# Channel attention and a gated feed-forward: steps of 1024 tokens (and one of 896 per batch) in place of 752

## The chip, the cores and the metric

The kernel runs on one core of one Trainium2 chip. The metric is the device time of one execution in microseconds; the median of several runs is compared.

## The reference

Two computations in sequence, all in float32. `q`, `k` and `v` have the shape (2, 6016, 256), `w_in` (256, 2048), `w_out` (2048, 256).

```
qn = q / (norm(q, axis=1) + 1e-06);  kn = k / (norm(k, axis=1) + 1e-06)
s = kn.transpose(0, 2, 1) @ qn / tau          # 256 x 256 for each batch
a = softmax(s, axis=-1)
x = v @ a                                     # 12032 tokens x 256
h = x @ w_in
g = h * (1.0 / (1.0 + exp(-h)))
out = g @ w_out
```

## The kernel before

**Head.** For each batch, 47 rows of 128 tokens of `q` and `k` are loaded in chunks of up to 3 rows into a ring of 9 slots (`load_chunk`, L222; two of the slots lie in `wp_raw0`, L118). PE sums the scores of all tokens (`score_chunk`, L336), ACT squares and DVE adds the squares (L503, L680), `sum_norms` (L341) sums them over the partitions. Softmax gives `probs`. Then `fold` (L359) multiplies `probs` into `w_in` once for each batch, so that the tokens of `v` go through one folded matrix to the hidden layer.

**Two-part numbers.** Every matrix factor is held as a rounded part and its rest (`_hi`, `_lo`, type float32r), and a product is three matmuls: hi by hi, hi by lo, lo by hi (`product`, L370, lines 373 to 375; `output_part`, L405, lines 408 to 410; `fold`, lines 365 to 367).

**Steps.** The tokens of a batch are cut into 8 steps of 2 x 376 (TOK = 376), 16 steps in all. The hidden layer of a step is a 2 x 2 block product for each of 8 pairs of 128-wide blocks of `d_ff`, done with 7 products in place of 8: factors A12, A22, A11 and the sums S1 to S4 of the folded matrix, and B11, B21, B22 with the sums T1 to T4 of the token halves. A pair is 7 x 3 product matmuls and 8 x 3 output matmuls, 45 in all, each over TOK columns. PE's order within a pair is written out by hand (`step`, L433): four first products (P1, P6, P5, P7), the first outputs of the pair before, three last products (P2, P3, P4), the last outputs of the pair before. Between them ACT copies P1 into `u` (L575), DVE adds the partial sums (L773, L777, L780, L792, L794), ACT applies silu (L588, L591, L601) and rounds (L595, L560), DVE subtracts for the rests (L796, L766). All of these cover TOK or 2 x TOK elements of each partition. Each engine works its list strictly in order and waits on semaphores.

**Tokens of the next step.** SP loads four blocks of `v` into `v_raw` (`load_v`, L232) once the split of the step before is over (`next_v`, L264). DVE makes T1 to T4 into `t_raw` after pairs 1 to 3 (`sum_v`, L739), ACT rounds B in pair 2 and T in pair 4 (L551, L555), DVE splits after pairs 4 to 6 (`split_v`, L752). `b_hi` and `b_lo` are double buffers. For step 0 POOL makes the sums and splits during the head (L307 to L321).

**Factors.** In step 0, PE also folds the second batch into `wp_raw1` (in pair 0, four folds after the first products, four after the last), and ACT and DVE round and split the factors of the first batch two pairs ahead (`round_a`, `sum_a`, `split_a`). The last step of batch 0 and the first of batch 1 replace them by those of batch 1 (`reloading`, L786 to L789).

**Outputs.** They are summed over the 8 pairs in four PSUM banks. ACT copies them in pair 0 of the next step into `out_sb`, a tile of its own (`copy_out`, L562), after the store of the step before has landed; SP stores each half (`store`, L258), and its order alternates stores and loads:

```
                    store(2 * it + half - 1)
                    next_v(0, 2 * it + half)
```

## Time and profile before

| | |
|---|---|
| median of 3 runs | 1106.34 us (1106.28 to 1107.59) |
| profiled execution, its own time | 1107.88 us |
| its span, first to last instruction | 1106.1 us |
| mean granted TensorE clock | 1.000 |
| busy: PE, DVE, ACT, POOL | 99%, 67%, 58%, 3% |
| step matmuls | 5760 of 376 columns |

The profile is one execution. PE is TensorE's matmuls, PEld its weight loads, DVE VectorE, ACT ScalarE, POOL GpSimd, SP the engine that issues most transfers. Matmuls are pipelined and the profile models their ends, so what one matmul costs is read from start to start. A row such as L373 names the line of the kernel printed above.

### The profile page before, as it was taken

The page shows a single profiled execution, that of the slowest core. Times are in us where ns is not written, and L with a number is a line of the kernel's source. Part 1 is how long each engine was busy: PE and PEld are TensorE (multiplying, and loading weights), DVE is VectorE, ACT ScalarE, POOL GpSimd, SP SyncE. Part 2 cuts the span into 40 slices and gives each one's busy share as a digit, 9 for nine tenths or more (in the row PEclk, how much of TensorE's full clock was granted, in tenths as well). Part 3 has the DMA queues.
Part 4 walks back from the last instruction along what each step waited for, and adds up shares of the span by engine and source line. Part 5 has one row for each costly group of instructions (what it writes and reads, how often), then busy time and mean ns, then how long its engine had stood idle before and what let it go on. Part 6 is the DMA issues. An engine that isn't in the chain of part 4 may idle for free.

```text
span 1106.1 us, 16838 instructions
## 1 busy us (share of the span) xinstructions
PE 1099.7 (99%) x6264; PEld 1082.7 (98%) x6264; DVE 741.2 (67%) x1194; ACT 646.0 (58%) x977; POOL 32.4 (3%) x24
## 2 busy tenths in 40 slices
PE   9999999999999999999999999999999999999998
PEld 7888999999999999999999999999999999999998
DVE  5686796666666666666687776666666666666654
ACT  5786765555555555555565656555554655555544
POOL 2450000000000000000000000000000000000000
PEclk9999999999999999999999999999999999999999
DMA  9990001010101001010100000010100000010000
GB/s 344 394 363 1 1 1 57 1 56 1 29 29 29 28 14 42 0 56 0 31 25 28 29 29 29 1 57 1 57 1 28 28 28 28 0 56 0 28 0 28
DMA packets 30627, 54.12 MB, mean 49 GB/s; under 512 B 2928, under 2 KB 22128, under 8 KB 30576
## 3 DMA queue, kind: packets, MB, share of 16 engines
q1 hardware_dynamic: 30000, 52.83, 13.5%
q10 hardware_dynamic: 576, 0.66, 0.2%
q8 instruction: 26, 0.43, 0.2%
q14 instruction: 25, 0.20, 0.1%
HBM read 41.16 MB, written 12.32 MB: 48 GB/s over the span
## 4 chain that ended last, share of the span: by engine, by line
PE 94%; DMA 2%; ACT 2%; DVE 1%; issue 1%; SPq 0%; ACTq 0%; DVEq 0%
PE ps_o L410 16%; PE ps_o L409 16%; PE ps_o L408 16%; PE ps_h L373 14%; PE ps_h L375 14%; PE ps_h L374 14%; PE ps_o L336 3%; DMA qk<-k_dram 2%; ACT ps_h L503 1%; DVE square_sum L680 0%; PE ps_h L365 0%; PE ps_h L366 0%; PE ps_h L367 0%; PE ps_o L366 0%; PE ps_o L367 0%
## 5 line engine op out<-in xcount | busy, mean ns | idle before, releaser
L373 PE MATMUL ps_h<-b_hi,a_hi_rest 128*128 128x376 f32 x672 | 223.9, 333 | 0.0
L375 PE MATMUL ps_h<-b_hi,a_lo_rest 128*128 128x376 f32 x672 | 223.9, 333 | 0.0
L374 PE MATMUL ps_h<-b_lo,a_hi_rest 128*128 128x376 f32 x672 | 223.3, 332 | 0.0
L792 DVE TENSOR_TENSOR h_b<-ps_h,u 128x376 f32<-128x376 f32 x128 | 70.4, 550 | 164.4 <-PE ps_h L375 164.2
L410 PE MATMUL ps_o<-g_hi_b,wo_lo 128*128 128x376 f32 x512 | 171.4, 335 | 0.0
L773 DVE TENSOR_TENSOR u<-ps_h,u 128x376 f32<-128x376 f32 x128 | 70.3, 550 | 150.8 <-ACT u L575 136.6
L409 PE MATMUL ps_o<-g_lo_b,wo_hi 128*128 128x376 f32 x512 | 171.2, 334 | 0.0
L408 PE MATMUL ps_o<-g_hi_a,wo_hi 128*128 128x376 f32 x512 | 170.8, 334 | 0.0
L410 PE MATMUL ps_o<-g_hi_a,wo_lo 128*128 128x376 f32 x512 | 170.8, 334 | 0.0
L408 PE MATMUL ps_o<-g_hi_b,wo_hi 128*128 128x376 f32 x512 | 170.6, 333 | 0.0
L409 PE MATMUL ps_o<-g_lo_a,wo_hi 128*128 128x376 f32 x512 | 170.4, 333 | 0.0
L591 ACT ACTIVATE h_a<-ps_h 128x376 f32<-128x376 f32 x128 | 62.1, 485 | 150.1 <-PE ps_h L375 150.1
L601 ACT ACTIVATE h_b<-h_b 128x752 f32<-128x752 f32 x128 | 106.8, 835 | 41.3 <-DVE h_b L794 41.3
L588 ACT ACTIVATE h_a<-h_a 128x376 f32<-128x376 f32 x128 | 66.3, 518 | 107.1 <-DVE h_a L780 105.7
L575 ACT ACTIVATE u<-ps_h 128x376 f32<-128x376 f32 x128 | 62.1, 485 | 114.2 <-PE ps_h L375 114.1
L374 PEld LDWEIGHTS ps_h<-b_lo,a_hi_rest 128*128 128x128 f32 x672 | 126.5, 188 | 0.0
L375 PEld LDWEIGHTS ps_h<-b_hi,a_lo_rest 128*128 128x128 f32 x672 | 126.2, 188 | 0.0
L373 PEld LDWEIGHTS ps_h<-b_hi,a_hi_rest 128*128 128x128 f32 x672 | 126.1, 188 | 0.0
L796 DVE TENSOR_TENSOR g_lo_a<-h_a,g_hi_a 128x752 fp32r<-128x752 f32 x128 | 119.3, 932 | 1.8 <-ACT g_hi_a L595 1.8
L766 DVE TENSOR_TENSOR g_lo_b<-h_b,g_hi_b 128x752 fp32r<-128x752 f32 x128 | 119.3, 932 | 1.6 <-ACT g_hi_b L560 1.6
L595 ACT ACTIVATE g_hi_a<-h_a 128x752 fp32r<-128x752 f32 x128 | 106.8, 834 | 7.2
L560 ACT ACTIVATE g_hi_b<-h_b 128x752 fp32r<-128x752 f32 x128 | 105.7, 826 | 0.7 <-PE ps_o L410 0.7
(111 smaller groups left out, 1752.8 us busy)
## 6 DMA issues: line engine op xcount, KB each, us to landing
v_raw<-v_t_dram SPq DMA_DIRECT2D x64, 188.0 KB, 2.7
out_t_dram<-out_sb SPq DMA_DIRECT2D x30, 376.0 KB, 2.8
qk<-q_dram SPq DMA_DIRECT2D x23, 384.0 KB, 9.3
qk<-k_dram SPq DMA_DIRECT2D x23, 384.0 KB, 12.3
wp_raw<-q_dram SPq DMA_DIRECT2D x6, 384.0 KB, 9.1
wp_raw<-k_dram SPq DMA_DIRECT2D x6, 384.0 KB, 10.7
wp_raw<-w_out_dram SPq DMA_DIRECT2D x4, 512.0 KB, 12.2
wp_raw<-w_in_dram SPq DMA_DIRECT2D x4, 512.0 KB, 13.1
```

What stands on the lines that cost most here:

```text
L373: nc.tensor.matmul(ps_h[:, bank, 0:TOK], w_hi, x_hi, start=start, stop=False, skip_group_check=True)
L374: nc.tensor.matmul(ps_h[:, bank, 0:TOK], w_hi, x_lo, start=False, stop=False, skip_group_check=True)
L375: return nc.tensor.matmul(ps_h[:, bank, 0:TOK], w_lo, x_hi, start=False, stop=stop, skip_group_check=True)
L408: nc.tensor.matmul(out, wo_hi[:, block_, d], g_hi[:, i, :], start=start, stop=False)
L409: nc.tensor.matmul(out, wo_hi[:, block_, d], g_lo[:, i, :], start=False, stop=False)
L410: return nc.tensor.matmul(out, wo_lo[:, block_, d], g_hi[:, i, :], start=False, stop=stop)
L560: nc.scalar.activation(g_hi_b[:], h_b[:], ACT.Copy).then_inc(hi_b, 1)
L595: nc.scalar.activation(g_hi_a[:], h_a[:], ACT.Copy).then_inc(hi_a, 1)
L601: nc.scalar.activation(h_b[:], h_b[:], ACT.Silu).then_inc(silu_b, 1)
L766: nc.vector.tensor_tensor(g_lo_b[:], h_b[:], g_hi_b[:].bitcast(F32), ALU.subtract).then_inc(lo_b, 1)
L792: nc.vector.tensor_tensor(h_b[:, 0, :], ps_h[:, BANK_P5, 0:TOK], u[:], ALU.add).then_inc(c12_made, 1)
L796: nc.vector.tensor_tensor(g_lo_a[:], h_a[:], g_hi_a[:].bitcast(F32), ALU.subtract).then_inc(lo_a, 1)
```

## The change

The tokens of a batch go in five steps of 2 x 512 and a last one of 2 x 448 (6 steps for each batch, 12 in all). Matmuls of the last step cover 448 columns; elementwise instructions cover 512 in all steps. To hold the wider tiles: `out_sb` becomes a view of `v_raw`; T3 and T4 are written over `v_raw`'s first and third block, so `t_raw` has two blocks; `b_lo1` takes the place of `wp_raw0`, and the factor order T1 to B22 lets each part of it be written after the pairs that it covers are used up; four ring slots lie in that region; `probs` and `q_scale` move to the area shared by early and late tiles. The order on SP is now, for each step: both stores, a wait for their landing, then the load of the step after the next, written out instead of looped. `copy_out` waits for the split of the next tokens rather than for a store. Sums, roundings and splits of tokens are regrouped over pairs 2 to 6. In the head, fold 0 of the first batch is placed before `sum_norms(1)`, and its copy before the second batch's roots; ACT rounds the first tokens in three pieces. The loops of PE, ACT and DVE now run over an odd and an even step, with steps 0, 5, 6 and 11 written out.

```diff
-TOK = 376
+TOK = 512
+NARROW = 448
...
-B11, B21, B22, T1, T2, T3, T4 = range(7)
+T1, T2, T3, T4, B11, B21, B22 = range(7)
...
-    STEPS = N // (2 * TOK)
+    WIDE = N // (2 * TOK)
+    STEPS = WIDE + 1
...
+        with ExitStack() as early:
+            wp_raw = [sb("wp_raw0", [P, PAIRS, 4, P], stack=early)]
+            homes = [sb(f"home{n}", [P, slot + C], stack=early)[:, 0:slot] for n in range(2)]
+        b_lo1 = sb("b_lo1", [P, FACTORS, TOK], F32R)
+        sb("rest_of_wp_raw0", [P, (4 * PAIRS * P - FACTORS * TOK)])
...
-        t_raw = sb("t_raw", [P, 4, TOK])
+        out_sb = v_raw[:].rearrange("p (t c) n -> p t c n", c=CK)
+        t_raw = sb("t_raw", [P, 2, TOK])
         b_hi = [sb("b_hi0", [P, FACTORS, TOK], F32R)]
-        b_lo = [sb("b_lo0", [P, FACTORS, TOK], F32R)]
+        b_lo = [sb("b_lo0", [P, FACTORS, TOK], F32R), b_lo1]
...
@@ sync, load_v and the stores
-                sp.dma_start(v_raw[:, 0, :], v_halves[:, b, 0, 2 * step + 1, :]).then_inc(v_loaded, 16)
-                sp.dma_start(v_raw[:, 1, :], v_halves[:, b, 0, 2 * step, :]).then_inc(v_loaded, 16)
-                sp.dma_start(v_raw[:, 2, :], v_halves[:, b, 1, 2 * step, :]).then_inc(v_loaded, 16)
-                sp.dma_start(v_raw[:, 3, :], v_halves[:, b, 1, 2 * step + 1, :]).then_inc(v_loaded, 16)
+            def load_v(step):
+                first, n = tokens_of(step)
+                for i, (c, t) in enumerate(((0, 1), (0, 0), (1, 0), (1, 1))):
+                    sp.dma_start(v_raw[:, i, 0:n], v_t[step // STEPS, c * P:(c + 1) * P,
+                                                       first + t * n:first + (t + 1) * n]).then_inc(v_loaded, 16)
...
+            def out_half(step, t):
+                first, n = tokens_of(step)
+                first += step // STEPS * N + t * n
+                return out_t.rearrange("(c p) n -> p c n", p=P)[:, :, first:first + n]
+            for step in range(ALL - 1):
+                n = tokens_of(step)[1]
+                for late, t in enumerate((1, 0)):
+                    sp.wait_ge(out_copied, 2 * step + late + 3)
+                    sp.dma_start(out_half(step, t), out_sb[:, t, :, 0:n]).then_inc(out_stored, 16)
+                if step < ALL - 2:
+                    sp.wait_ge(out_stored, 32 * step + 64)
+                    load_v(step + 2)
+            for late, t in enumerate((1, 0)):
+                last = out_half(ALL - 1, t)
+                sp.wait_ge(last_copied_dve, late + 1)
...
@@ gpsimd, step 0: the same new order of sums and splits
...
@@ tensor
-                nc.tensor.matmul(ps_h[:, bank, 0:TOK], w_hi, x_hi, start=start, stop=False, skip_group_check=True)
...
+                x_hi, x_lo = b_hi[par][:, t, 0:n], b_lo[par][:, t, 0:n]
+                nc.tensor.matmul(ps_h[:, bank, 0:n], w_hi, x_hi, start=start, stop=False, skip_group_check=True)
+                nc.tensor.matmul(ps_h[:, bank, 0:n], w_hi, x_lo, start=False, stop=False, skip_group_check=True)
+                return nc.tensor.matmul(ps_h[:, bank, 0:n], w_lo, x_hi, start=False, stop=stop,
                                         skip_group_check=True)
-            def first_products(n, pair, par, folded=False):
+            def first_products(n, pair, par, tok, folded=False):
...
-            sum_norms(1)
             pe.wait_ge(w_in_split, PARTS)
             pe.wait_ge(probs_split, 1)
+            pe.wait_ge(chunk_added, 2 * len(CHUNKS) - 1)
             for group in range(FOLDS):
                 fold(0, group)
+                if group == 0:
+                    sum_norms(1)
...
             step(0, 0, opening=True)
-            step(1, 1)
-            with pe.Fori(1, STEPS // 2) as it:
-                step(2 * it, 0)
+            with pe.Fori(0, WIDE // 2) as it:
                 step(2 * it + 1, 1)
-            step(STEPS, 0, reloaded=True)
-            step(STEPS + 1, 1)
-            with pe.Fori(STEPS // 2 + 1, ALL // 2) as it:
-                step(2 * it, 0)
+                step(2 * it + 2, 0)
+            step(STEPS - 1, 1, tok=NARROW)
+            step(STEPS, 0, before=NARROW, reloaded=True)
+            with pe.Fori(STEPS // 2, ALL // 2 - 1) as it:
                 step(2 * it + 1, 1)
-            first_outputs(PAIRS * ALL - 1, ALL - 1, PAIRS - 1)
+                step(2 * it + 2, 0)
...
@@ scalar
+            def round_t12(it, par):
+                act.wait_ge(t12_summed, it + 1)
+                nc.scalar.activation(b_hi[par][:, T1:T2 + 1, :], t_raw[:], ACT.Copy).then_inc(t12_rounded, 1)
             def round_v(it, par):
                 act.wait_ge(v_loaded, 64 * it + 64)
-                nc.scalar.activation(b_hi[par][:, B11:B22 + 1, :], v_raw[:, 1:4, :], ACT.Copy).then_inc(v_rounded, 1)
-            def round_t(it, par):
-                act.wait_ge(v_summed, it + 1)
-                nc.scalar.activation(b_hi[par][:, T1:T4 + 1, :], t_raw[:], ACT.Copy).then_inc(v_rounded, 1)
+                nc.scalar.activation(b_hi[par][:, B11:B22 + 1, :], v_raw[:, 1:4, :], ACT.Copy).then_inc(b_rounded, 1)
+            def round_t34(it, par):
+                act.wait_ge(t4_summed, it + 1)
+                nc.scalar.activation(b_hi[par][:, T3:T4 + 1, :], v_raw[:, 0:3:2, :], ACT.Copy).then_inc(t34_rounded, 1)
             def round_b(n):
...
+                act.wait_ge(v_split, 3 * it + 6)
+                nc.scalar.activation(out_sb[:, 1], ps_o[:, CK:2 * CK, :], ACT.Copy).then_inc(out_copied, 1)
                 act.wait_ge(o2_done, PAIRS * it + PAIRS + 1)
-                nc.scalar.activation(out_sb[:, 0], ps_o[:, 0:CK, 0:TOK], ACT.Copy).then_inc(out_copied, 1)
+                nc.scalar.activation(out_sb[:, 0], ps_o[:, 0:CK, :], ACT.Copy).then_inc(out_copied, 1)
             def step(it, par, opening=False, reloading=None, closing=False):
                 for pair in range(PAIRS):
...
+                    if not closing and pair == 3:
+                        round_t12(it + 1, 1 - par)
+                    if not closing and pair == 4:
                         round_v(it + 1, 1 - par)
-                    if not closing and pair == 4:
-                        round_t(it + 1, 1 - par)
+                    if not closing and pair == 6:
+                        round_t34(it + 1, 1 - par)
                     act.wait_ge(c22_made, n + 1)
                     nc.scalar.activation(h_a[:, 0, :], h_a[:, 0, :], ACT.Silu).then_inc(silu_22, 1)
                     act.wait_ge(p2_done, n + 1)
                     act.wait_ge(lo_a, n + 1)
-                    nc.scalar.activation(h_a[:, 1, :], ps_h[:, BANK_P1, 0:TOK], ACT.Silu).then_inc(silu_11, 1)
+                    nc.scalar.activation(h_a[:, 1, :], ps_h[:, BANK_P1, :], ACT.Silu).then_inc(silu_11, 1)
                     act.wait_ge(silu_22, n + 1)
...
+                if g == SECOND + 3:
+                    round_t12(0, 0)
                 if g == SECOND + 4:
                     root_norms(0)
                 if g == SECOND + 5:
                     exponentials(0)
-                    round_t(0, 0)
+                    round_t34(0, 0)
                 if g in (25, 26, 27, 28):
                     round_w_in(g - 25)
                 if g == SECOND + 13:
                     round_probs(0)
...
@@ vector
+            def sum_t123(it):
+                dve.wait_ge(v_loaded, 64 * it + 64)
+                dve.wait_ge(v_split, 3 * it)
+                nc.vector.tensor_tensor(t_raw[:, 0, :], b12_raw, b11_raw, ALU.subtract).then_inc(v_step, 1)
+                dve.wait_ge(v_step, it + 1)
+                nc.vector.tensor_tensor(b12_raw, b22_raw, b12_raw, ALU.subtract)
+                nc.vector.tensor_tensor(t_raw[:, 1, :], b22_raw, t_raw[:, 0, :], ALU.subtract).then_inc(t12_summed, 1)
+            def sum_t4(it):
+                dve.wait_ge(v_split, 3 * it + 2)
+                dve.wait_ge(t12_summed, it + 1)
+                nc.vector.tensor_tensor(b21_raw, b21_raw, t_raw[:, 1, :], ALU.subtract).then_inc(t4_summed, 1)
+            def split_t12(it, par):
+                dve.wait_ge(t12_rounded, it + 1)
+                nc.vector.tensor_tensor(b_lo[par][:, T1:T2 + 1, :], t_raw[:], b_hi[par][:, T1:T2 + 1, :].bitcast(F32),
+                                        ALU.subtract).then_inc(v_split, 1)
+            def split_v(it, par):
+                dve.wait_ge(b_rounded, it + 1)
+                nc.vector.tensor_tensor(b_lo[par][:, B11:B22 + 1, :], v_raw[:, 1:4, :],
+                                        b_hi[par][:, B11:B22 + 1, :].bitcast(F32), ALU.subtract).then_inc(v_split, 1)
+            def split_t34(it, par):
+                dve.wait_ge(t34_rounded, it + 1)
+                nc.vector.tensor_tensor(b_lo[par][:, T3:T4 + 1, :], v_raw[:, 0:3:2, :],
+                                        b_hi[par][:, T3:T4 + 1, :].bitcast(F32), ALU.subtract).then_inc(v_split, 1)
             def split_b(n):
...
-                    if not closing and 1 <= pair <= 3:
-                        sum_v(it + 1, pair - 1)
-                    if not closing and 4 <= pair <= 6:
-                        split_v(it + 1, 1 - par, pair - 4)
+                    if not closing and pair == 2:
+                        sum_t123(it + 1)
+                    if not closing and pair == 3:
+                        split_t12(it + 1, 1 - par)
+                    if not closing and pair == 5:
+                        split_v(it + 1, 1 - par)
+                        sum_t4(it + 1)
+                    if not closing and pair == 6:
+                        split_t34(it + 1, 1 - par)
...
```

## Rows read from the trace of the kernel before

**Rows 1.** The page: busy time by engine, 40 slices of the span, the chain.

```profile
PE 1099.7 (99%) x6264; PEld 1082.7 (98%) x6264; DVE 741.2 (67%) x1194; ACT 646.0 (58%) x977; POOL 32.4 (3%) x24
...
DVE  5686796666666666666687776666666666666654
...
GB/s 344 394 363 1 1 1 57 1 56 1 29 29 29 28 14 42 0 56 0 31 25 28 29 29 29 1 57 1 57 1 28 28 28 28 0 56 0 28 0 28
...
PE 94%; DMA 2%; ACT 2%; DVE 1%; issue 1%; SPq 0%; ACTq 0%; DVEq 0%
```

**Rows 2.** Windows view; us, busy us (x instructions) by engine, granted clock, DMA share, GB/s.

```profile
103.70:1102.70 999.00, 999.00 (x5808) 996.50 (x5807) 667.53 (x1090) 571.21 (x870) 0.00 (x0) 1.00 0.07 23
```

**Rows 3.** The groups of instructions by form, for the step matmuls on PE.

```profile
L373 PE MATMUL ps_h<-b_hi,a_hi_rest 128*128 128x376 f32 x672 | 223.9, 333 | 0.0
```

**Rows 4.** Timeline of one pair, in time: start us, us, engine, line, [idle before].

```profile
500.68 0.33 PE L373 MATMUL ps_h<-b_hi,a_hi_rest 128*128 128x376 f32 x1
...
502.22 0.33 PE L408 MATMUL ps_o<-g_hi_b,wo_hi 128*128 128x376 f32 x1
...
505.58 0.55 DVE L773 TENSOR_TENSOR u<-ps_h,u 128x376 f32<-128x376 f32 x1 [1.31 <-ACT u L575]
...
507.22 0.93 DVE L766 TENSOR_TENSOR g_lo_b<-h_b,g_hi_b 128x752 fp32r<-128x752 f32 x1
...
508.40 0.33 PE L373 MATMUL ps_h<-b_hi,a_hi_rest 128*128 128x376 f32 x1
```

**Rows 5.** Timeline of PE: score matmuls, then folds of 512 columns.

```profile
19.83 4.48 PE L336 MATMUL ps_o<-wp_raw 128*128 128x256 f32 x20
...
92.30 0.40 PE L366 MATMUL ps_h<-w_in_lo,probs_hi 128*128 128x512 f32 x1
...
98.84 0.40 PE L367 MATMUL ps_h<-w_in_hi,probs_lo 128*128 128x512 f32 x1
...
105.87 0.39 PE L365 MATMUL ps_o<-w_in_hi,probs_hi 128*128 128x512 f32 x1
...
111.14 0.39 PE L367 MATMUL ps_o<-w_in_hi,probs_lo 128*128 128x512 f32 x1
...
112.90 0.40 PE L365 MATMUL ps_o<-w_in_hi,probs_hi 128*128 128x512 f32 x1
...
118.18 0.39 PE L367 MATMUL ps_o<-w_in_hi,probs_lo 128*128 128x512 f32 x1
```

**Rows 6.** Timeline of the head, rows of ACT, DVE and PE.

```profile
53.09 1.14 ACT L551 ACTIVATE b_hi<-v_raw 128x1128 fp32r<-128x1128 f32 x1
...
56.76 1.59 ACT L503 ACTIVATE ps_h<-qk 128x768 f32<-128x768 f32 x2 [0.38 <-DMA qk<-k_dram]
...
65.75 1.44 ACT L555 ACTIVATE b_hi<-t_raw 128x1504 fp32r<-128x1504 f32 x1
...
87.71 1.81 DVE L680 TENSOR_TENSOR square_sum<-ps_h,square_sum 128x768 f32<-128x768 f32 x2
...
91.12 0.67 PE L344 MATMUL ps_o<-square_sum,ones 128*128 128x256 f32 x2 [1.02 <-DVE square_sum L686]
```

**Rows 7.** The groups by form again, for elementwise durations.

```profile
L796 DVE TENSOR_TENSOR g_lo_a<-h_a,g_hi_a 128x752 fp32r<-128x752 f32 x128 | 119.3, 932 | 1.8 <-ACT g_hi_a L595 1.8
...
L792 DVE TENSOR_TENSOR h_b<-ps_h,u 128x376 f32<-128x376 f32 x128 | 70.4, 550 | 164.4 <-PE ps_h L375 164.2
...
L755 DVE TENSOR_TENSOR b_lo<-v_raw,b_hi 128x1128 fp32r<-128x1128 f32 x15 | 19.9, 1326 | 0.0
...
L543 ACT ACTIVATE wo_hi<-wp_raw 128x1024 fp32r<-128x1024 f32 x4 | 4.2, 1043 | 0.0
```

**Rows 8.** Transfers of v_raw (tile view), then those issued by L262 (line view).

```profile
DMA to landing us min/median/max: 2.3/2.7/11.0
...
DMA to landing us min/median/max: 2.5/2.8/4.7
```

**Rows 9.** Timeline of the tail on PE.

```profile
1100.71 0.44 PE L408 MATMUL ps_o<-g_hi_b,wo_hi 128*128 128x376 f32 x1
```

More of the change, by code:

```diff
@@ L271, in _ @@
-            with sp.Fori(1, STEPS // 2 - 1) as it:
-                for half in range(2):
-                    store(2 * it + half - 1)
-                    next_v(0, 2 * it + half)
-            for n in range(STEPS - 2, STEPS):
-                store(n - 1)
-                next_v(1, n)
-            with sp.Fori(STEPS // 2, ALL // 2 - 1) as it:
-                for half in range(2):
-                    store(2 * it + half - 1)
-                    next_v(1, 2 * it + half)
-            for n in range(ALL - 3, ALL - 1):
-                store(n)
@@ L400, in last_products @@
                 pe.wait_ge(u5_made, n + 1)
[L401 removed]
+                product(pair, par, tok, BANK_P5, S4, B22, False, True).then_inc(p3_done, 1)
                 pe.wait_ge(c22_made, n + 1)
[L403 to L405 removed]
+                product(pair, par, tok, BANK_P7, A22, T4, False, True).then_inc(p4_done, 1)
@@ L413, in output, with first_outputs @@
+            def output(block_, half, g_hi, g_lo, i, tok, start, stop):
                 for c in range(CK):
-                    mm = output_part(block_, half, g_hi, g_lo, i, c, start, stop)
+                    mm = output_part(block_, half, g_hi, g_lo, i, c, tok, start, stop)
                 return mm
-            def first_outputs(n, it, pair):
+            def first_outputs(n, it, pair, tok):
                 pe.wait_ge(lo_a, n + 2)
@@ L440, in step @@
                         pe.wait_ge(a_split, PAIRS + pair + 1)
-                    first_products(n, pair, par, folded=(opening and pair == 0))
+                    first_products(n, pair, par, tok, folded=(opening and pair == 0))
                     if opening and pair == 0:
@@ L455, in step @@
                     else:
-                        last_outputs(n - 1, (pair - 1) % PAIRS)
+                        last_outputs(n - 1, (pair - 1) % PAIRS, tok if pair else before)
             for free in (o1_done, o2_done):
@@ L628, in _ @@
                     round_probs(0)
+            copy_folded(0, 0)
             root_norms(1)
             nc.scalar.activation(scratch[:], ones[:, 0:1], ACT.Exp)
-            for group in range(3):
+            for group in range(1, 3):
                 copy_folded(0, group)
```

196 lines of the change are left out of this document (74 added, 122 removed).

## The prediction

> **What bounds the kernel now.** I read the page first. PE is busy for 99% of the span and holds 94% of the chain of work that ended last, while DVE and ACT are far from full [rows 1]. A busy PE need not be at its peak, so the next view is one stretch of the windows: from the first product of step 0 (103.70) to the last output matmul (1102.70) PE starts 5808 matmuls in 999.0 us, with a granted clock of 1.00 (the 2.4 GHz level) [rows 2]. Of these, 48 are the folds of the second batch; the other 5760 are 16 steps x 8 pairs x 45 matmuls of 376 columns. Nothing in this stretch waits for data: a pair that starts at 500.68 is followed by the next at 508.40, 7.72 us for 45 matmuls, **171.6 ns from start to start** [rows 4]. (The 333 ns in the group's row is the modelled length of one, which overlaps its neighbour's [rows 3]; it isn't what one costs.) 376 columns at 2.4 GHz are 156.7 ns, so each matmul costs 14.8 ns beyond its columns. Over the stage: 999.0 us less 48 x 229.4 ns = 11.0 us for the folds (priced below) is 988.0 us, or 171.5 ns for each of 5760. The stage is 89% of the span; what happens to the time is decided by what a matmul of another width costs.
>
> **The change, part by part.**
>
> *Fewer, wider matmuls.* 6016 tokens of a batch become five steps of 2 x 512 and one of 2 x 448: 10 wide and 2 narrow steps in all, 3600 matmuls of 512 columns and 720 of 448, 4320 in place of 5760. The columns stay the same: 3600 x 512 + 720 x 448 = 5760 x 376 = 2,165,760, or 902.4 us at 2.4 GHz. Only what lies beyond the columns can change. The trace has matmuls of the same type at 512 columns, the folds, at two prices [rows 5]. The folds of the second batch run inside step 0: 105.87 to 111.14 is 23 intervals in 5.27 us, 229.1 ns; 112.90 to 118.18 is 23 in 5.28 us, 229.6 ns. Those of the first batch run before the steps: 92.30 to 98.84 is 28 intervals in 6.54 us, 233.6 ns. So a 512-wide matmul costs 229.4 or 233.5 ns, 16.1 or 20.2 ns beyond its columns. I take 229.4: these folds lie between the 376-wide products, and, like the steps, they alternate with other tiles and have ACT and DVE at work beside them. For 448 columns no row exists; on the line from 171.5 (376) to 229.4 (512) it is 202.2 ns.
> Sum: 3600 x 229.4 = 825.8 us, 720 x 202.2 = 145.6 us, together 971.4 us against 988.0: **-16.6 us**.
> Ends: with 233.5 ns, and 204.4 for 448 on its line, it is 840.6 + 147.2 = 987.8 us, no gain at all. At the other end, if the extra stays at the 14.8 ns of the present stage, 3600 x 228.1 + 720 x 201.5 = 966.2 us, -21.8. A smaller extra exists in the trace (20 score matmuls of 256 columns in fp32, two passes each: (4.48 - 0.38) / 19 = 215.8 ns, 2.5 beyond 512 cycles [rows 5]), but the folds are the same type as the steps and show 16 at the very width in question, which excludes it as more than a far end (-75 us).
>
> *The rule that speaks against this.* The rows say that one matmul less, at equal columns, is worth about 15 ns. The Trainium skill, "TensorE: Matmul & The Clock Gate", section "Back-to-back issue gap", puts a warm matmul at its columns over 2.4 GHz plus about 2.5 ns, so that by it the 1440 matmuls less would be worth 3.6 us. The fp32 score rows agree with it (2.5 ns), the steps and the folds don't (14.8 and 16 to 20 ns); what the rest of their cost is, fixed or by the column, it doesn't say.
>
> *Elementwise work of the steps.* It lies beside PE; what hides it is the pair's length, which goes from 7.72 to 45 x 0.2294 = 10.3 us (x 1.34). DVE's 376-wide operations go from 550 to about 688 ns (the line through 550 at 376 and 932 at 752), its 752-wide ones from 932 to about 1215 [rows 7]. Per pair 5 x 0.69 + 2 x 1.22 = 5.9 us of 10.3, where it was 4.6 of 7.7: more room, not less. ACT grows by less than x 1.34 likewise. The narrow steps keep 512-wide elementwise work under pairs of 45 x 0.202 = 9.1 us: 5.9 of 9.1, still room. Today PE comes to the late outputs, which read what L766 makes, at 502.22 + 7.72 = 509.94, and L766 ends at 508.15, so 1.8 us is the slack that has to last [rows 4]. With these durations laid out by hand in a wide pair (products 0.69 each, outputs 1.38 for each six), split_b ends some 5.1 us into it and is read at 7.6: 2.5 us of slack. Cost 0.
>
> *Token parts.* Three sums now stand in one pair (3 x 0.69 = 2.1 us on DVE) and one pair has split_v with the fourth sum (1536 wide, 1.75, and 0.69: 2.4 us), where one insert was 1.33 at most (L755 [rows 7]). DVE's wait before the next pair's first sum is 1.31 us in the row shown [rows 4], and in a wide pair by the same layout 2.3 us (9.9 to 12.2). So the longest insert delays `u` by 0.1 us, against PE's 2.5. ACT's inserts (1.04, 1.5, 1.04) stand ahead of `silu_22`, whose result is wanted 3 us later. The DVE row of the page is fullest near the opening step [rows 1], where folded factors are split too; there DVE's base of 4.6 of 7.7 becomes 5.9 of 10.3, and the factor work stays what it is, so the opening is relieved. Cost 0; without cover, an insert costs its excess, some 0.5 us for each step.
>
> *Outputs in the tokens' tile.* copy_out now waits until the next tokens are split, which is one pair before it is reached: nothing. The load of step n+2 is queued on SP behind both stores of step n and their landing. Into a wide step: second copy done at about 11.6 us (late outputs of the pair before, then 1.1 us), 0.4 issue, store landed 2.8 to 4.7 us later, four load issues 1.8 us, landed 2.7 us on (a third more bytes: say 3.7) [rows 8]; tokens stand at 20 to 22 us. DVE asks for them after pair 2, at 30 us. Cost 0, with 8 us in hand; even the longest load of the trace, 11.0 us, lands by 30. Nothing else of SP waits behind it but the next stores, a step later.
>
> *The head.* DMA feeds it till 56.76, then ACT [rows 6]. The first tokens are 1 MB in place of 0.75, at 363 GB/s [rows 1] 0.7 us more ahead of the later chunks. ACT's three roundings are 1.5 + 1.04 + 1.04 against 1.14 + 1.44: +1.0 us, the first of them partly in its waits for DMA. I put +1.0 us on the head (0 if all hides, +1.7 if nothing does). POOL's sums take a third longer, and their consumers come 8 us later. Against it, fold 0 no longer waits for the last norms: it starts after the first of DVE's last two additions (87.71 + 0.9) instead of after sum_norms, which starts at 91.12 and takes 0.9, so its 1.4 us leave the path: -1.4 us. Net **-0.4**. The other seven folds still cover the exponentials; if not, up to 1 us comes back.
>
> *The tail.* The last split waits on elementwise work 1024 wide. Today PE starts the last outputs at 1100.71 [rows 9], some 0.1 us later than its pace would have it; the chain c21, silu, rounding, split grows by about 1.0 us and PE's cover by 24 matmuls x 30 ns = 0.7. With a wider last copy and store: **+0.3**.
>
> Sum: -16.6 - 0.4 + 0.3 = -16.7 us. The profiled execution took 1107.9 us, 1.5 above the median, so it would come out at 1091.2; the median goes from 1106.3 to **1089.6 us**.
>
> **Rivals.**
> 1. *The extra goes with the columns* (0.12). For it: 233.5 / 171.5 = 1.361, and 512 / 376 = 1.362, a striking match. Against it: 44 later intervals at 229.4 under the conditions nearest to the steps. Stage 987.8, with head and tail -0.3 us: 1106.0, no change.
> 2. *Most of the extra goes by columns and 2.5 ns by the matmul* (0.07). 1440 x 2.5 ns = 3.6 us off: 1106.3 - 3.6 - 0.1 = 1102.6. Its fixed part is what the fp32 score rows show; the Trainium skill's page named above gives the same number as a rule.
> 3. *Elementwise work peeps out* (0.05): the doubled inserts of the token parts or the factors' steps cost PE 0.5 to 1 us a step, 12 steps, so 6 to 12 us: 1096 to 1102. Against it: no wait of PE in the present stage.
> 4. *The shared tile makes every step wait* (0.08). Store landing, load issue and load stand in one chain, where the load was free to start half a step ahead. It decides from some 32 us into a step (DVE's 30 plus PE's 2); from 33.7 us on, 1.7 us on each of 10 steps, it eats the 16.7 us. At 35 us PE stands 3 us a step, 30 in all: 1120, slower. Against it: 20 to 22 us by the rows; for it, only that loads of 11.0 us occur, in the head.
>
> **How the numbers follow.** The forecast, 229.4 give or take the folds' spread of 1.5 ns (x 4320 = 6.5 us) and the 1 us terms, has 0.68: 1082 to 1096. Rivals 2 and 3 take it to 1103. Rival 1 and rival 4 (0.20) are left outside: range 1082 to 1103. Faster by over 0.2% (2.2 us, about what a measurement of this kernel can tell from no change): 0.68 + 0.07 + 0.05 = 0.80; within it 0.12; slower 0.08.
>
> **What would show it.** Right: 45 matmuls from pair to pair in about 10.3 us in wide steps and 9.1 in narrow ones; the first product of step 0 at about 103.3; no PE wait for DVE or DMA at step borders; DVE's wait for tokens after pair 2 absent. Wrong: pairs of 10.51 us (rival 1) or 10.47 (rival 2), weight loads of the products and outputs idle until DVE releases them (rivals 3 and 4), tokens landing later than 30 us into a step (rival 4).

## The result, and the profile after

The changed kernel takes **1080.84 us** (median of 6 runs, 1080.67 to 1082.6) against 1106.31 (6 runs, 1105.86 to 1107.59) of the kernel before on the same chip: ratio 0.977, 95% interval 0.9757 to 0.9782. Faster, as forecast, but by 25.5 us where 16.7 were forecast, and 1.2 us below the low end of the range. The profiled execution took 1080.67 us with a span of 1078.6.

The page of the changed kernel, the lines that answer to [rows 1]:

```profile
PE 1072.0 (99%) x4824; PEld 905.4 (84%) x4824; DVE 724.1 (67%) x942; ACT 622.9 (58%) x781; POOL 35.6 (3%) x24
...
DVE  5777588567567566566688777567566566566665
...
GB/s 337 392 402 21 1 1 1 78 1 1 79 1 1 78 0 0 73 0 0 79 1 1 74 1 1 79 1 1 79 1 0 78 0 0 73 0 1 39 1 34
...
PE 93%; DMA 3%; ACT 2%; DVE 1%; issue 1%; SPq 0%; ACTq 0%; DVEq 0%
```

1440 matmuls are gone and PE is as full as before. The one share that moved much is PEld's, from 98% to 84%. The Trainium skill, "Perfetto Trace Analysis", section "Identifying the Most-Contended Engine", has a reader judge the headroom of TensorE by the arithmetic done against the peak and by the busy share of its weight loads. Here the second of these fell while nothing came free. The windows view of the changed kernel shows it, for the stage from the first product of step 0 to the last output matmul, which answers to [rows 2]:

```profile
102.06:1075.11 973.05, 973.01 (x4368) 819.66 (x4367) 649.45 (x838) 547.69 (x674) 0.00 (x0) 1.00 0.07 23
```

A weight load lasts 188 ns (819.66 us / 4367), and a slot (the time from one matmul's start to the next) is now longer than that. By this view PE still has no gap but for 0.04 us, at a granted clock of 1.00 (2.4 GHz). The span shrank by 27.5 us: **25.95 in the stage** (999.0 to 973.05), 1.64 ahead of it (103.70 to 102.06), and -0.1 behind it (3.4 us before, 3.5 now). The median shrank by less, because the profiled execution of the kernel before took 1.5 us more than its median.

What one matmul costs is read from start to start, in the timeline of PE. The first product of one pair and of the next, in a wide step and in a narrow one (L381 to L383 are now the products, L416 to L418 the outputs); [rows 4] is the answer of before:

```profile
301.32 0.39 PE L381 MATMUL ps_h<-b_hi,a_hi_rest 128*128 128x512 f32 x1
...
311.52 0.39 PE L381 MATMUL ps_h<-b_hi,a_hi_rest 128*128 128x512 f32 x1
...
534.38 0.36 PE L381 MATMUL ps_h<-b_hi,a_hi_rest 128*128 128x448 f32 x1
...
543.50 0.36 PE L381 MATMUL ps_h<-b_hi,a_hi_rest 128*128 128x448 f32 x1
```

45 matmuls in 10.20 us are **226.7 ns** for 512 columns, 13.3 beyond the columns' 213.3; 9.12 us are 202.7 for 448, 16.0 beyond. The forecast was 229.4 and 202.2. The second batch's folds, next to the products, cost 226.7 as well, where before they cost 229.4 [rows 5]: 104.80 to 110.01 is 23 intervals in 5.21 us.

The head, in the timeline of PE, against [rows 6]:

```profile
89.03 0.58 PE L373 MATMUL ps_h<-w_in_hi,probs_hi 128*128 128x512 f32 x1
...
91.08 0.67 PE L352 MATMUL ps_o<-square_sum,ones 128*128 128x256 f32 x2 [0.31 <-DVE square_sum L705]
...
102.06 0.40 PE L381 MATMUL ps_h<-b_hi,a_hi_first 128*128 128x512 f32 x1
```

Fold 0 starts ahead of the norms, and from the norms to the first product it takes 10.98 us, where it took 12.58 (91.12 to 103.70).

Elementwise work, in the groups by form, against [rows 7]:

```profile
L818 DVE TENSOR_TENSOR g_lo_a<-h_a,g_hi_a 128x1024 fp32r<-128x1024 f32 x96 | 116.9, 1218 | 1.6 <-ACT g_hi_a L615 1.6
...
L814 DVE TENSOR_TENSOR h_b<-ps_h,u 128x512 f32<-128x512 f32 x96 | 66.4, 692 | 166.8 <-PE ps_h L383 166.6 <-issue 0.2
...
L778 DVE TENSOR_TENSOR b_lo<-v_raw,b_hi 128x1536 fp32r<-128x1536 f32 x11 | 19.3, 1752 | 0.0
```

And the shared tile in one step, in the timelines of SP and DVE. This step's first product is at 301.32 - 3 x 10.20 = 270.72:

```profile
281.18 1.39 SPq L285 DMA_DIRECT2D out_t_dram<-v_raw  x2
285.76 1.78 SPq L253 DMA_DIRECT2D v_raw<-v_t_dram  x4
...
300.54 0.69 DVE L761 TENSOR_TENSOR t_raw<-v_raw 128x512 f32<-128x512 f32 x1
...
302.95 0.69 DVE L795 TENSOR_TENSOR u<-ps_h,u 128x512 f32<-128x512 f32 x1 [0.40 <-PE ps_h L383]
```

The loads are out at 287.54 and land 3.7 us later (the page's median), about 291, 20.5 us into the step. DVE asks for them at 29.8 without a wait before it, and after the three sums it still waits for PE, not PE for it. The tail is the one place where PE now waits inside the stage, in its timeline:

```profile
1072.36 0.37 PE L418 MATMUL ps_o<-g_hi_a,wo_lo 128*128 128x448 f32 x1
1072.76 0.48 PE L416 MATMUL ps_o<-g_hi_b,wo_hi 128*128 128x448 f32 x1
1073.07 0.37 PE L417 MATMUL ps_o<-g_lo_b,wo_hi 128*128 128x448 f32 x1
```

Two slots take 0.71 us in place of 0.41. The 0.3 us are for the last split, `g_lo_b`, as the weight load ahead of the second one shows:

```profile
1072.76 0.19 PEld L416 LDWEIGHTS ps_o<-g_hi_b,wo_hi 128*128 128x128 f32 x1 [0.41 <-DVE g_lo_b L788]
```

### The profile page after: what moved, and what is told of

Its sections match the earlier page's. It is cut to its first block, busy times and chain, and to the rows that moved or that the text cites. A ratio compares the mean times of both kernels' runs of the same rounds, so it can differ in the third digit from the quotient of the medians.

```text
span 1078.6 us, 12988 instructions
## 1 busy us (share of the span) xinstructions
PE 1072.0 (99%) x4824; PEld 905.4 (84%) x4824; DVE 724.1 (67%) x942; ACT 622.9 (58%) x781; POOL 35.6 (3%) x24
## 4 chain that ended last, share of the span: by engine, by line
PE 93%; DMA 3%; ACT 2%; DVE 1%; issue 1%; SPq 0%; ACTq 0%; DVEq 0%
PE ps_o L416 16%; PE ps_o L418 16%; PE ps_o L417 16%; PE ps_h L383 14%; PE ps_h L381 14%; PE ps_h L382 14%; DMA qk<-k_dram 2%; ACT ps_h L515 2%; PE ps_o L344 1%; DMA wp_raw<-k_dram 1%; DVE square_sum L699 0%; PE ps_o L375 0%; PE ps_o L374 0%; PE ps_o L373 0%; PE ps_h L373 0%
## 5 line engine op out<-in xcount | busy, mean ns | idle before, releaser
L383 PE MATMUL ps_h<-b_hi,a_lo_rest 128*128 128x512 f32 (+1 forms) x504 | 194.1, 385 | 0.0
L382 PE MATMUL ps_h<-b_lo,a_hi_rest 128*128 128x512 f32 (+1 forms) x504 | 194.1, 385 | 0.0
L381 PE MATMUL ps_h<-b_hi,a_hi_rest 128*128 128x512 f32 (+1 forms) x504 | 194.0, 385 | 0.0
L416 PE MATMUL ps_o<-g_hi_b,wo_hi 128*128 128x512 f32 (+1 forms) x384 | 148.0, 385 | 0.0
L417 PE MATMUL ps_o<-g_lo_a,wo_hi 128*128 128x512 f32 (+1 forms) x384 | 147.9, 385 | 0.0
L418 PE MATMUL ps_o<-g_hi_b,wo_lo 128*128 128x512 f32 (+1 forms) x384 | 147.9, 385 | 0.0
L416 PE MATMUL ps_o<-g_hi_a,wo_hi 128*128 128x512 f32 (+1 forms) x384 | 147.9, 385 | 0.0
L417 PE MATMUL ps_o<-g_lo_b,wo_hi 128*128 128x512 f32 (+1 forms) x384 | 147.8, 385 | 0.0
L418 PE MATMUL ps_o<-g_hi_a,wo_lo 128*128 128x512 f32 (+1 forms) x384 | 147.8, 385 | 0.0
L818 DVE TENSOR_TENSOR g_lo_a<-h_a,g_hi_a 128x1024 fp32r<-128x1024 f32 x96 | 116.9, 1218 | 1.6 <-ACT g_hi_a L615 1.6
L381 PEld LDWEIGHTS ps_h<-b_hi,a_hi_rest 128*128 128x128 f32 x504 | 94.6, 188 | 17.6
L383 PEld LDWEIGHTS ps_h<-b_hi,a_lo_rest 128*128 128x128 f32 x504 | 94.6, 188 | 17.6
## 6 DMA issues: line engine op xcount, KB each, us to landing
wp_raw<-q_dram SPq DMA_DIRECT2D x8, 384.0 KB, 11.1
```

What stands on the lines that cost most here:

```text
L381: nc.tensor.matmul(ps_h[:, bank, 0:n], w_hi, x_hi, start=start, stop=False, skip_group_check=True)
L382: nc.tensor.matmul(ps_h[:, bank, 0:n], w_hi, x_lo, start=False, stop=False, skip_group_check=True)
L383: return nc.tensor.matmul(ps_h[:, bank, 0:n], w_lo, x_hi, start=False, stop=stop, skip_group_check=True)
L416: nc.tensor.matmul(out, wo_hi[:, block_, d], g_hi[:, i, 0:tok], start=start, stop=False)
L417: nc.tensor.matmul(out, wo_hi[:, block_, d], g_lo[:, i, 0:tok], start=False, stop=False)
L418: return nc.tensor.matmul(out, wo_lo[:, block_, d], g_hi[:, i, 0:tok], start=False, stop=stop)
```

## The experiments

Two explanations stood for the 2.7 ns that a wide matmul is cheaper than forecast. Either the width sets the extra (and the folds of before had paid for something else), or what sets it is where the tiles lie: the change also moved every tile that a matmul streams. In the kernel before, their rows of 376 floats have a stride of 1504 bytes, so that they begin at many remainders; now the stride is 2048 bytes and they begin alike, at the same remainder by 512 bytes as the weights. The recorded expectations call the first "theory width" and the second "theory layout"; "theory grid" is a later form of the second, in which the price moves in steps.

**w1_widths**: the changed kernel with each PE step cut to fewer columns, tiles left where they are.

```diff
-                step(2 * it + 1, 1)
-                step(2 * it + 2, 0)
+                step(2 * it + 1, 1, tok=480, before=384)
+                step(2 * it + 2, 0, tok=384, before=480)
...
-                step(2 * it + 1, 1)
-                step(2 * it + 2, 0)
+                step(2 * it + 1, 1, tok=416, before=376)
+                step(2 * it + 2, 0, tok=376, before=416)
...
```

> The changed kernel, but PE's steps cover other widths at the same tiles: 384 columns in even steps of batch 0, 480 in its odd steps, 448 in its last; 376 and 416 in batch 1, 448 in its last. The columns beyond are not computed, so outputs are left out. Theory layout (the extra beyond N/2.4 GHz depends on where the tiles lie, which all start at one remainder by 512 bytes): the extra is 13 to 14 ns at every width, so 376 costs 170, 384 173.4, 416 186.7, 480 213.4. Theory width (the extra depends on the number of columns): 376 costs 171.5 again as in the kernel before, 448 203, and the others lie between, with 512 a favourable width of its own. Fixed 14.8 ns for all would give 384 174.8, 416 188.1, 480 214.8.

Pairs in its timeline of PE, of 384, 480 and 416 columns:

```profile
150.98 0.33 PE L381 MATMUL ps_h<-b_hi,a_hi_rest 128*128 128x384 f32 x1
...
158.78 0.33 PE L381 MATMUL ps_h<-b_hi,a_hi_rest 128*128 128x384 f32 x1
...
200.16 0.37 PE L381 MATMUL ps_h<-b_hi,a_hi_rest 128*128 128x480 f32 x1
...
209.90 0.38 PE L381 MATMUL ps_h<-b_hi,a_hi_rest 128*128 128x480 f32 x1
...
763.52 0.35 PE L381 MATMUL ps_h<-b_hi,a_hi_rest 128*128 128x416 f32 x1
...
772.00 0.35 PE L381 MATMUL ps_h<-b_hi,a_hi_rest 128*128 128x416 f32 x1
```

Over 45 intervals each: 173.3, 216.4 and 188.4 ns; over all pairs of such a step 173.3, 216.7 and 188.3. With the 512 of the changed kernel and the 376-wide steps (173.3), the scan at one placement is

```
columns            376    384    416    448             480    512
ns start to start  173.3  173.3  188.3  202.7 or 206.7  216.7  226.7
beyond columns      16.6   13.3   15.0   16.0 or 20.0    16.7   13.3
```

The 448-wide matmuls have two prices, in the same kernel and with the same tiles in the same places. The rows show 45 intervals in the last step of batch 0, then 45 in the last step of batch 1:

```profile
489.62 0.37 PE L381 MATMUL ps_h<-b_hi,a_hi_rest 128*128 128x448 f32 x1
...
498.74 0.37 PE L381 MATMUL ps_h<-b_hi,a_hi_rest 128*128 128x448 f32 x1
...
887.76 0.37 PE L381 MATMUL ps_h<-b_hi,a_hi_rest 128*128 128x448 f32 x1
...
897.06 0.37 PE L381 MATMUL ps_h<-b_hi,a_hi_rest 128*128 128x448 f32 x1
```

That is 9.12 us and 9.30 us for 45 matmuls, at a granted clock of 1.00 in both. The step of batch 0 began at the higher price too, and went over to 202.7 ns at 482 us, where PE waited twice for 0.1 us. So the placement doesn't settle the price by itself; what else does is not known.

From 384 to 512 columns the slot rises by 53.4 ns, which is 128 columns at 2.4 GHz to the tenth: **the extra is paid per matmul, not by the column**. Rivals 1 and 2 of the prediction both need it to grow with the width; they are out. It isn't constant either: within one placement it moves by 3.4 ns, and with the higher price of 448 by 6.7, and not in the order of the widths. Of the two theories neither holds as written: the one extra of 13 to 14 ns (layout) is met at 384 and 512 alone, and 376 columns cost 173.3 and not 171.5 (width). (The 939.5 us have no use as a time: besides the lighter PE, 512-wide elementwise work is too long for the narrowest pairs.)

**s1_shift192**: the changed kernel with all weight tiles (`wo`, `a_hi`, `a_lo`) moved by 192 bytes against the streamed ones. The program is the same instruction for instruction; only unused tiles are put between.

```diff
+        sb("pad0", [P, 48])
...
+        sb("pad1", [P, 80])
...
+            sb("pad2", [P, 48], stack=early)
...
```

> The changed kernel with all weight tiles (wo, a_hi, a_lo) moved by 192 bytes against the moving tiles. Theory layout: 512-wide matmuls of the steps go from 226.7 to 229 to 233 ns as in the folds of the kernel before, whose tiles also stood 192 bytes apart, so the stage gets 8 to 24 us longer and the time is 1089 to 1105 us. Theory width or traffic: 226.7 stays, 1080.8 us.

1087.48 us (one run): 228.9 ns at 512 columns, 200.0 at 448. Its stage in the windows view:

```profile
102.88:1081.98 979.10, 979.03 (x4368) 819.73 (x4367) 650.24 (x838) 547.58 (x673) 0.00 (x0) 1.00 0.07 23
```

979.1 against 973.05 us: placement alone costs 2.2 ns a wide matmul and gives 2.7 back at a narrow one. In this relation of tiles, 192 bytes apart as in the folds of the kernel before, a 512-wide matmul costs nearly the 229.4 ns that the prediction took from those folds, and the whole kernel nearly the 1089.6 us that it forecast.

**h1_norms_first**: the changed kernel with the last norms ahead of fold 0, as before.

```diff
+            sum_norms(1)
...
-                if group == 0:
-                    sum_norms(1)
...
-            copy_folded(0, 0)
-            for group in range(1, 3):
+            for group in range(3):
```

> The changed kernel with the head's order undone: sum_norms(1) before fold 0 and its copy after the roots. Expected: first product of step 0 at 103.4 to 103.7 instead of 102.06, time 1082.2 us (+1.4). If the head's gain came from elsewhere, 1080.8.

1082.63 us (one run); the stage is 973.05 again. Its timeline of PE:

```profile
91.96 0.67 PE L352 MATMUL ps_o<-square_sum,ones 128*128 128x256 f32 x2 [2.13 <-DVE square_sum L702]
...
104.31 0.40 PE L381 MATMUL ps_h<-b_hi,a_hi_first 128*128 128x512 f32 x1
```

From the norms to the first product it takes 12.35 us against 10.98: the order is worth **1.4 us**. The rest of the 2.25 us between the two kernels is the arrival of the norms (91.96 against 91.08), which scatters by itself: in the traces of this study it lies between 89.8 and 92.4.

**p1_stride384**: the kernel *before*, 376 columns, with each row of the token and silu tiles padded to 384 floats, so that they all begin alike too, as in the changed kernel.

```diff
+STRIDE = 384
...
+        def sbt(name, shape, dt=F32, stack=ctx):
+            tile = sb(name, shape[:-1] + [STRIDE], dt, stack)
+            return tile[(slice(None),) * (len(shape) - 1) + (slice(0, TOK),)]
...
-        b_hi = [sb("b_hi0", [P, FACTORS, TOK], F32R)]
+        b_hi = [sbt("b_hi0", [P, FACTORS, TOK], F32R)]
...
```

> The kernel before, 376 columns, with the token tiles held at a stride of 384 elements, so that all tiles of products, outputs and folds start at one remainder by 512 bytes, as in the changed kernel. Same work. Theory layout: 171.5 ns goes to about 170.1 (13.4 extra), the stage gets 8 us shorter, 1098 us, and the folds of batch 1 go from 229.3 to 226.7. Theory width: 171.5 and 1106.3 us stay; folds 226.7 only if their own rate hangs on layout.

1117.22 us (4 runs, 1116.83 to 1117.6), ratio 1.0099 (1.0082 to 1.0116) to the kernel before, which took 1106.11 beside it: slower by 11.1 us with the same program. A matmul costs 173.3 ns where it cost 171.5; that is also what 376 columns cost in w1. Both theories missed: one had 8 us less, the other no change. So beginning alike is not what makes a matmul cheap at every width.

The next questions are how far placement reaches, whether the narrow steps can be made cheaper, and when the shared tile would bite.

**s2_shift64_128** and **s3_shift256_384**: as s1, with `wo` moved by 64 and `a` by 128 bytes, and by 256 and 384.

```diff
+        sb("pad0", [P, 16])
...
+        sb("pad1", [P, 112])
...
+            sb("pad2", [P, 32], stack=early)
...
```

> The changed kernel with wo_hi and wo_lo moved by 64 bytes against the moving tiles, and a_hi and a_lo by 128. Theory grid: the groups of output matmuls and of product matmuls take constant patterns between 226.7 (two steps, the floor) and 233.3 ns (three); if the period is 256 bytes or less, one of them is like the shift by 192. No group falls under 226.7. Theory width: all stay at 226.7.

> The changed kernel with wo_hi and wo_lo moved by 256 bytes and a_hi and a_lo by 384. Theory grid: with a period of 256 bytes the outputs stay at 226.7, and the products are as with 128 bytes; nothing under 226.7. Theory width: all stay at 226.7.

1103.63 and 1101.28 us, one run each: the same kernel, nearly as slow as the one before. The same 300 us of the windows view, first of the changed kernel:

```profile
200.00:500.00 300.00, 300.00 (x1325) 248.43 (x1324) 193.50 (x234) 163.20 (x196) 0.00 (x0) 1.00 0.08 28
```

of s2:

```profile
200.00:500.00 300.00, 300.00 (x1290) 242.22 (x1289) 186.80 (x227) 159.62 (x192) 0.00 (x0) 1.00 0.08 28
```

and of s3:

```profile
200.00:500.00 300.00, 300.00 (x1296) 243.41 (x1295) 188.02 (x228) 160.43 (x192) 0.00 (x0) 1.00 0.08 28
```

PE is without a gap in all three at the same clock, and starts 1325, 1290 or 1296 matmuls of 512 columns. In ns from start to start: 226.7; 232.9 for products and outputs alike; 233.5 for the products and 230.4 for the outputs. So the extra of a 512-wide matmul ran from 13.3 to 20.2 ns, and the time by up to 22.8 us. The outputs of s3 were expected to stay at 226.7, since `wo` moved by 256 bytes; they didn't.

**n1_offsets**: the narrow steps use columns 16 to 463 of their tiles in the first batch, and 64 to 511 in the second, in place of 0 to 447.

```diff
+PLACE = [slice(16, 16 + NARROW), slice(64, 64 + NARROW)]
...
-                x_hi, x_lo = b_hi[par][:, t, 0:n], b_lo[par][:, t, 0:n]
+                x_hi, x_lo = b_hi[par][:, t, n], b_lo[par][:, t, n]
...
```

> The changed kernel with the 448 columns of a narrow step placed in the middle of their 512-wide tiles: from column 16 (64 bytes) in batch 0, from column 64 (256 bytes) in batch 1. Theory grid (a matmul costs its columns, two steps of 6.67 ns, and a rest under one step that hangs on how the tiles lie to each other, with a period of 256 bytes or less): the first goes from 202.7 to 200.0 ns, as when the weights were moved by 192 bytes, the second stays at 202.7; time 1 us less. Theory width (448 costs 202.7 wherever it lies, and 200.0 came from another cause): both stay at 202.7 and the time at 1080.8.

Windows of n1, in the narrow step of the first batch, and then of the changed kernel:

```profile
530.00:600.00 70.00, 70.00 (x348) 64.81 (x347) 59.32 (x88) 45.83 (x59) 0.00 (x0) 1.00 0.06 21
```

```profile
530.00:600.00 70.00, 70.00 (x344) 64.28 (x343) 58.57 (x86) 45.97 (x59) 0.00 (x0) 1.00 0.05 16
```

Column 16 gives 200.2 ns, column 64 the old 202.7. In time (1080.27, 4 runs, 1079.22 to 1080.64; ratio 0.9758, 0.9742 to 0.9775) a gain of 0.9 us is too small to be seen, but the spacing shows it: 64 bytes at the start of an operand change what a matmul costs. (The columns written in PSUM move along here. In s1 nothing moves but the weights, and 448 columns come to 200.0.)

**d1_late_tokens**: SP holds the next tokens back, in the first batch until the third pair's first product is through, in the second one pair longer.

```diff
                     sp.wait_ge(out_stored, 32 * step + 64)
+                    sp.wait_ge(p1_done, PAIRS * (step + 1) + (3 if step + 1 < STEPS else 4))
                     load_v(step + 2)
```

> The changed kernel with the load of the next tokens held back: in batch 0 until the first product of pair 2 is done (21 us into a step, tokens there at about 27), in batch 1 until that of pair 3 (31 us, tokens at about 37). Theory cover (the shared tile costs nothing as long as tokens stand at 30 us, DVE's sum after pair 2): batch 0 unchanged to 1 us, batch 1 some 3 to 5 us of PE idle in each wide step that loads, 12 to 25 us in all, 1093 to 1106 us. If the shared tile had cost something already, batch 0 gets longer as well, by some us for each step.

1111.26 us, one run, span 1108.1. In the first batch, with tokens some 27 us into the step, PE is untouched: 1776 matmuls from 118 to 520 us, as without the edit. In the second batch, in its list of waits (us in total, how many, the longest):

```profile
DVE t_raw L762 <- DMA v_raw<-v_t_dram: 36.5, 5, 7.4
...
PEld ps_h L382 <- DVE h_a L800: 20.7, 5, 4.2
```

One of these steps has its first product at 588.49; DVE asks at 617.85 (29.4 us into it) and gets its tokens at 625.20. Being 7.35 us late costs PE 4.2, so the point from which it decides is about 29.4 + 3.2 = 32.6 us. Five waits of up to 4.2 us are 20.7 us, but the span grew by 29.5, more than the 12 to 25 that were expected. The rest is in the stretch behind each wait, here in the windows and the timeline of PE behind the first:

```profile
624.50:628.50 4.00, 0.33 (x2) 0.00 (x0) 3.23 (x5) 1.06 (x1) 0.00 (x0) 0.90 0.01 6
628.60:634.00 5.40, 5.40 (x13) 4.24 (x14) 5.33 (x10) 3.43 (x5) 0.00 (x0) 0.50 0.00 0
634.00:640.00 6.00, 6.00 (x27) 4.94 (x26) 3.64 (x5) 4.27 (x6) 0.00 (x0) 0.95 0.01 3
```

```profile
629.62 0.63 PE L384 MATMUL ps_h<-b_hi,a_lo_rest 128*128 128x512 f32 x1
...
633.88 0.63 PE L417 MATMUL ps_o<-g_hi_b,wo_hi 128*128 128x512 f32 x1
```

After 4 us without work the granted clock is 0.50 (1.2 GHz). Matmuls start slowly for 3.0 to 6.1 us behind the five waits, in one of them only after the first few; 10 intervals in 4.26 us are 426 ns. The Trainium skill, "TensorE: Matmul & The Clock Gate", section "Wait — 56ns, not 53.3ns?", has a 512-column matmul at 426.7 ns at the lower clock and at 215.7 at the upper one. The first number this trace bears out, with no extra at all beyond 512 columns / 1.2 GHz; the second it doesn't (226.7 at best).

Last, a version that uses this, and the two kernels on equal terms.

**v1_best**: the narrow steps at column 16 in both batches, and the last step's elementwise work on 448 columns in place of 512. **a2_after** is the changed kernel again, beside it.

```diff
+PLACE = [slice(16, 16 + NARROW)] * 2
...
-            split_b(PAIRS * ALL - 1)
+            split_b(PAIRS * ALL - 1, PLACE[1])
```

> The changed kernel with the narrow columns at 16 to 464 of their tiles in both batches, and the elementwise work of the last step on these 448 columns alone. Theory grid: narrow matmuls cost 200.2 ns in both (2.5 ns x 720 = 1.8 us), the two late matmuls of the tail lose their wait (0.3 us): 1078.7 us against 1080.8 of the changed kernel. If only the tail counts: 1080.5.

> The changed kernel itself, beside the version above on the same chip: 1080.8 us, ratio to the kernel before 0.977; 226.7 and 203.1 ns per matmul, the first product of step 0 at 102 to 103.

1079.14 us (5 runs, 1078.73 to 1080.93; ratio 0.9762, 0.9749 to 0.9776) against 1080.49 (5 runs, 1079.9 to 1081.74; ratio 0.977, 0.9756 to 0.9783). The stage is 971.1 us against 973.0: 720 x 2.5 ns = 1.8 us from the narrow steps, 0.2 from the tail, whose two slots take 0.50 us now. The intervals of the ratios overlap, so the gain of 1.35 us rests on the traces more than on the times.

**p2_before_shift64**: p1 with the streamed tiles moved by 64 bytes against the weights.

```diff
+        sb("pad0", [P, 16])
         v_raw = sbt("v_raw", [P, 4, TOK])
...
```

> The kernel before at a stride of 384 elements, with all moving tiles (tokens and silu parts) moved by 64 bytes against the weights, the relation that brought 448 columns to 200.0 to 200.2 ns. Theory grid: the 376-wide matmul takes a constant price between 170.0 (its 156.7 and two steps) and 176.7 (three); if it is near 170, the stage loses 8 us against the kernel before (1098 us) with no matmul less, and the tile positions alone would have been worth a third of the change. If the price doesn't move from the 173.3 of the aligned form, 1117 us.

1100.88 us (4 runs, 1100.62 to 1102.88), ratio 0.9959 (0.9944 to 0.9974): **64 bytes are 16.3 us** between p1 and p2, and the kernel before gets 5.3 us faster than the unpadded one beside it (1106.16) without a change to its program. The stage in the windows of p1, then of p2:

```profile
102.66:1112.05 1009.39, 1009.39 (x5809) 1007.12 (x5807) 667.81 (x1090) 571.51 (x870) 0.00 (x0) 1.00 0.07 23
```

```profile
102.22:1095.41 993.19, 993.19 (x5808) 990.67 (x5807) 666.80 (x1090) 570.56 (x870) 0.00 (x0) 1.00 0.07 23
```

1009.4 us at 173.3 ns and 993.2 at 170.5, against 999.0 at 171.5 without padding [rows 2]. The stage gave 5.8 us and not 8.

**s4_shift256_all**: the changed kernel with all weights moved by 256 bytes.

```diff
+        sb("pad0", [P, 64])
...
+        sb("pad1", [P, 64])
...
+            sb("pad2", [P, 64], stack=early)
...
```

> The changed kernel with all weight tiles (wo, a_hi, a_lo) moved by 256 bytes against the moving tiles, both by the same amount. If tile positions count only by their remainder by 256 bytes: 226.7 ns and 1080.8 us, like the changed kernel. If they count by 512 bytes or more, or if the gap between weights of products and of outputs matters too: another constant between 226.7 and 233.5 ns, 1080.8 to 1104 us, and the 230.4 of the mixed shift tells which.

1080.40 us (one run), with 226.7 and 202.7 ns: no different from the unshifted kernel. A shift common to all weights seems to count by its remainder to 256 bytes. s3, where `wo` is moved by 256 and `a` by 384, is slow for its outputs too, so the relation of `wo` to the streamed tiles isn't all that an output pays for. Either the two kinds of weights matter to each other, or what runs before a matmul does; no run tells these apart.

## Why the prediction was right in direction and short in size

- **What bounds the kernel**: right. PE has no gap in either stage but for the tail, and 94% of the gain is there.
- **Fewer, wider matmuls**: the mechanism is right, since the extra is paid per matmul and 1440 are gone. The sum was -16.6 us and the stage came out at -25.95. The step that failed is the choice of 229.4 ns for 512 columns: it measured 226.7, and 3600 x 2.7 = **9.7 us** is the difference. Against it, 448 columns cost 202.7 and not 202.2 (+0.4), the last split waits 0.3 inside the stage, and 48 folds at 226.7 give 0.1 back: -16.6 - 9.7 + 0.4 + 0.3 - 0.1 = -25.7, and rounding of the prices leaves 0.2. The far end of that sum had been worked out with 228.1, the present extra of 14.8 ns (-21.8 us); the extra came out at 13.3.
- **Why it failed**: a price of 512 columns was carried from one placement in SBUF to another. The prediction let the width alone decide what a matmul costs; the diff moved every streamed tile, and that edit was given no term. In the relation of tiles that the folds of the kernel before have (s1), a 512-wide matmul costs 228.9 ns; in the changed kernel's it costs 226.7, and in s2 and s3 230.4, 232.9 and 233.5, in kernels that differ only by unused bytes. Seen from here, the range for the stage should have run from 3600 x 226.7 to 3600 x 233.5, which is 24 us. The 1.5 ns that the prediction calls the folds' spread isn't in its rows either: the second batch's folds differ by 0.5 ns, and the two batches' by about 4.
- **The two fold prices** [rows 5] are not explained by placement. The folds of both batches read the same four tiles (`probs_hi`, `probs_lo`, `w_in_hi`, `w_in_lo`) in the same places, and cost 233.6 and 229.4 ns. They write other PSUM banks and have other work around them; no run separates these. The two prices of 448 columns in w1 (206.7 and 202.7) are the same kind of thing. The choice of the lower price by "the conditions nearest to the steps" was no more than plausible.
- **How the 25.95 us divide** into fewer matmuls and placement has no single answer, since the two act on each other. With all tiles beginning alike, the stage goes from 1009.4 (p1) to 973.05: 36.3 us, 25 ns for each of the 1440 matmuls less. With the streamed tiles 64 bytes on against the weights (in s1 the weights stand 192 bytes on, which is the same if only the remainder by 256 counts) it goes from 993.2 (p2) to 979.1: 14.1 us, 10 ns each. From the better placement of the one to the better of the other, it is 20.1 us, 14 ns each, and the 5.8 us from 999.0 to 993.2 are then placement. With s2's or s3's placement the whole change would have brought 3 to 5 us.
- **Elementwise work, token parts, opening**: right at cost 0. 0.692 and 1.218 us against 0.69 and 1.22, the long insert 1.752 against 1.75, and no wait of PE for DVE before the tail.
- **The shared tile**: right. Tokens stand at 20.5 us (20 to 22 forecast), are wanted at 29.8 (30); some 9 us in hand. Rival 4's point of decision, 32 us, measured 32.6 in d1; its price left out the slow clock behind each wait, 8.8 us in all on top of 20.7 in d1.
- **The head**: -0.4 forecast, -1.64 in the two traces. The order of fold 0 gives the 1.4 that were worked out (h1). The +1.0 for ACT and the larger tokens can't be seen: the norms came at 91.08 against 91.12, with a scatter of over 2 us from run to run. Whether it is 0 or 1.0 stays open.
- **The tail**: +0.3 forecast; 0.3 us of wait where there had been 0.1 [rows 9], and 0.1 behind the last matmul.
- **The rivals**: 1 and 2 fell with the pair of 10.20 us (they had 10.51 and 10.47), and w1 shows why. The striking ratio 233.5 / 171.5 was chance: it compares two placements, and a fold price that the same tiles didn't keep. 3 and 4 didn't occur. The later folds that stood against rival 1 are 46 intervals, not 44.
- **The rule weighed there**, of 2.5 ns beyond the columns: the Trainium skill, "TensorE: Matmul & The Clock Gate", section "Back-to-back issue gap", gives it as the gap of a matmul by itself, which the prediction leaves out. No placement tried came near it for these matmuls (13.3 at least). A cost per matmul is what the saving is made of, but at five times the size or more.

What stays open is the law behind the price. The runs show that a streamed operand's start against the weights' matters, and that 256 bytes common to all weights don't. They don't show why the extra differs between 384 and 376 or 448 columns, why the same tiles can have two prices, nor whether 13.3 ns is the floor. Beginning alike, 376 and 384 columns cost the same 173.3 ns, and a weight load takes 188, longer than that slot; whether the loads have a part in the price of the narrow matmuls was not tried.

## What to carry to other kernels

Price a matmul from start to start, and only from a row whose operands lie in SBUF as they will after the change; a change of tile shape is a change of placement, and gets a term and a range of its own. When PE is without a gap and still above columns over clock, shift the weight tiles by 64, 128 and 192 bytes with unused tiles before redesigning anything: here unused bytes alone moved the time by -5.3 us (p2 against the kernel before) to +22.8 us (s2 against the changed kernel). Fewer and wider matmuls gain about what one costs beyond its columns: 10 to 25 ns here for each that is gone, depending on the placement that they are compared at.

## What the runs showed of the hardware that was not expected

- A float32r matmul of 128 x 128 weights cost its columns at 2.4 GHz plus 13.3 to 20.2 ns, and this depended on where its operands lay: 64 bytes of padding changed 1117.2 us into 1100.9.
- Placement didn't settle it alone: in w1, 448 columns from the same tiles cost 206.7 ns in one stretch and 202.7 in another, and it changed over at two short waits of PE.
- At 1.2 GHz the extra was gone: 426 ns for 512 columns in d1.
- Waits of up to 4.2 us on PE cost more than themselves: 29.5 us of span for 20.7 us of waits in d1, with the granted clock at 0.50 behind each.
- A weight load takes 188 ns whether the slot has 171 or 233 ns, so that the share of PEld says how wide the matmuls are, and not how loaded PE is.
